# Attention preamble and first FFN tile: whole decay load, later bonus products, halved inverse scans, another order of DVE and ACT work

## The reference, cut

```python
def _attn_ref(r, k, v, w, u):              # B, H, S, D = 2, 8, 768, 48
    for t in range(S):
        kt, vt, rt, wt = (k[:, :, t], v[:, :, t], r[:, :, t], w[:, :, t])
        cur = np.einsum('bhd,bhe->bhde', u[None] * kt, vt)
        y[:, :, t] = np.einsum('bhd,bhde->bhe', rt, state + cur)
        state = wt[:, :, :, None] * state + np.einsum('bhd,bhe->bhde', kt, vt)
...
x = x @ w_in; x = where(x > 0, x, exp(min(x, 0)) - 1); x = x @ w_out    # 1536 x 384, 2048 wide
...
for e in range(4): out += p[:, e] * (relu(x @ w1[e]) @ w2[e])           # 1024 wide each
```

## Time and profile before

| | us |
|---|---|
| median of 3 runs | 662.99 (662.85 to 663.19) |
| the profiled execution, its own time | 663.25 |
| its span in the trace | 661.5 |
| PE busy in the span | 650.6 (98%) |
| DVE, ACT, POOL busy | 393.1, 238.0, 244.3 |

### The profile page before, as it was taken

One profiled execution on the slowest core, in us unless ns is written; L12 is line 12 of the kernel. 1 busy time (PEld: TensorE's weight loads), 2 busy tenths in 40 slices (PEclk: granted clock), 3 DMA queues, 4 the chain that ended last, 5 costly groups with the idle time before them and its releaser, 6 DMA issues.

```text
span 661.5 us, 12711 instructions
## 1 busy us (share of the span) xinstructions
PE 650.6 (98%) x4687; PEld 599.0 (91%) x4687; DVE 393.1 (59%) x717; ACT 238.0 (36%) x550; POOL 244.3 (37%) x292
## 2 busy tenths in 40 slices
PE   7998999999999999999999999999999999999998
PEld 5898999887778888999999999999999999999997
DVE  7878877765534333756565656565656565656563
ACT  4686655554445444422222222222222222222221
POOL 3898342221123079995007930008920009000000
PEclk9999999999999999999999999999999999999999
DMA  8923222220000033200002200003100011001011
GB/s 313 404 82 127 107 85 85 85 85 1 1 2 1 25 95 97 71 1 1 1 1 96 96 1 1 0 25 105 62 1 0 0 49 49 1 0 48 1 48 49
DMA packets 13423, 38.08 MB, mean 58 GB/s; under 512 B 1984, under 2 KB 4288, under 8 KB 13376
## 3 DMA queue, kind: packets, MB, share of 16 engines
q1 hardware_dynamic: 13088, 37.03, 16.0%
q10 hardware_dynamic: 288, 0.39, 0.2%
HBM read 35.06 MB, written 2.36 MB: 57 GB/s over the span
## 4 chain that ended last, share of the span: by engine, by line
PE 89%; DVE 3%; ACT 3%; issue 2%; DMA 1%; SPq 1%; DVEq 0%; ACTq 0%
PE bank L1143 28%; PE bank L1144 28%; PE bank L1145 28%; PE bank L1016 2%; DMA raw<-w_dram 1%; PE bank L1080 1%; ACT alpha L578 1%; PE bank L1039 1%; ACT neg L633 1%; PE bank L1027 1%; DVE st L784 1%; PE bank L1092 1%; ACT g_hi L641 0%; SPq L365 0%; DVE bank L845 0%
## 5 line engine op out<-in xcount | busy, mean ns | idle before, releaser
L1143 PE MATMUL bank<-x_lo,w_hi 128*128 128x256 f32 (+2 forms) x432 | 146.0, 338 | 0.9 <-DVE x_lo L809 0.9
L1145 PE MATMUL bank<-x_hi,w_hi 128*128 128x256 f32 (+2 forms) x432 | 143.3, 332 | 0.0
L1144 PE MATMUL bank<-x_hi,w_lo 128*128 128x256 f32 (+2 forms) x432 | 143.2, 331 | 0.0
L1144 PE MATMUL bank<-w_hi,g_lo 128*128 128x384 f32 x384 | 129.6, 338 | 0.0
L1145 PE MATMUL bank<-w_hi,g_hi 128*128 128x384 f32 x384 | 129.3, 337 | 0.0
L1143 PE MATMUL bank<-w_lo,g_hi 128*128 128x384 f32 x384 | 129.0, 336 | 0.0
L690 ACT ACTIVATE g_hi<-bank 128x512 fp32r<-128x512 f32 x96 | 57.6, 600 | 144.2 <-DVE bank L946 122.2
L1143 PEld LDWEIGHTS bank<-x_lo,w_hi 128*128 128x128 f32 x432 | 81.2, 188 | 10.0 <-POOL w_lo L470 1.0
L1145 PEld LDWEIGHTS bank<-x_hi,w_hi 128*128 128x128 f32 x432 | 81.2, 188 | 9.0
L1144 PEld LDWEIGHTS bank<-x_hi,w_lo 128*128 128x128 f32 x432 | 81.3, 188 | 8.3
L482 POOL TENSOR_TENSOR raw<-raw 128x128 f32<-128x128 f32 x16 | 7.4, 461 | 200.8 <-DMA raw<-w_dram 200.8
(11 more groups left out here) (111 smaller groups left out, 1146.1 us busy)
## 6 DMA issues: line engine op xcount, KB each, us to landing
raw<-w_dram SPq DMA_DIRECT2D x48, 384.0 KB, 3.6
rkw<-rkw_dram SPq DMA_DIRECT2D x10, 772.5 KB, 4.4
tok<-tok_dram SPq DMA_DIRECT2D x10, 576.0 KB, 6.1
out_dram<-acc SPq DMA_DIRECT2D x10, 192.0 KB, 1.9
rkw<-rkw_dram SPq DMA_DIRECT2D x2, 512.0 KB, 5.3
tok<-tok_dram SPq DMA_DIRECT2D x2, 192.0 KB, 5.5
out_dram<-acc ACTq DMA_DIRECT2D x2, 192.0 KB, 2.0
rkw<-rkw_dram SPq DMA_DIRECT2D x1, 260.5 KB, 5.2
```

Of the source, the lines that this page charges most:

```text
L1143: pe.matmul(out, wh, ml, start=start, stop=False, skip_group_check=shared)
L1144: pe.matmul(out, wl, mh, start=False, stop=False, skip_group_check=shared)
L1145: return pe.matmul(out, wh, mh, start=False, stop=stop, skip_group_check=shared)
```

## The change

- SP: the decays of chunk 0 come in one DMA, not in two halves; the two loads of u move ahead of the second decay load, and the constants behind it.
- DVE: the scan of chunk 0 is one instruction. `inverses(c)` for c >= 3 is cut into two halves of 260 columns, in steps 4c - 3 and 4c - 2, each between `elu` and `lo_g`. `add_update(c)` (c >= 2) goes from the end of step 4c + 3 to its beginning, ahead of `lo_x(c)`. The low part of slice 14 is made in steps 12 and 14, after `lo_g`.
- POOL: the product r*k of chunk 0 now waits for chunk 0's `scale_r`.
- ACT: `hi_x(1)` goes ahead of `hi_w(5)`; slice 6 is rounded inside step 0, the others follow a new table. `alphas`, `copy_tail`, `scale_state` come after the step's weight halves.
- PE: `values_odd(0)` goes ahead of `bonus(1)`.

```diff
-INVERSES = {c: step - 2 for c, step in SCORES.items()} | {FIRST: 3}
+INVERSES = {FIRST: 3}
+HALF_INVERSES = {c: step - 3 for c, step in SCORES.items() if c > FIRST}
...
-LO_BETWEEN = {1: (5, 0), 2: (5, 1), 3: (8, 0), 4: (8, 1), 6: (10, 0), 7: (10, 1), 14: (14, 1)}
-LO_AFTER = {10: (14, 0)}
+LO_BETWEEN = {1: (5, 0), 2: (5, 1), 3: (8, 0), 4: (8, 1), 6: (10, 0), 7: (10, 1)}
+LO_AFTER = {12: (14, 0), 14: (14, 1)}
...
-HI_FIRST = 7
-HI_BETWEEN = {0: ((7, 0), (7, 1)), 1: ((8, 0),), 2: ((8, 1),), 3: ((9, 0),), 4: ((9, 1),), 5: ((10, 0),), 6: ((10, 1),),
-              7: ((11, 0),), 8: ((11, 1), (12, 0)), 9: ((12, 1), (13, 0)), 10: ((13, 1), (14, 0)), 11: ((14, 1),),
-              12: ((15, 0),), 13: ((15, 1),)}
+HI_FIRST = 6
+HI_BETWEEN = {0: ((6, 0), (6, 1)), 1: ((7, 0),), 2: ((7, 1), (8, 0)), 3: ((8, 1),), 4: ((10, 0),), 5: ((10, 1),),
+              6: ((9, 0), (9, 1)), 7: ((11, 0),), 8: ((11, 1),), 9: ((12, 0), (12, 1)), 10: ((13, 0), (13, 1)),
+              11: ((14, 0), (14, 1)), 12: ((15, 0),), 13: ((15, 1),)}
...
-            load_decays(0, 0, SCAN // 2, s_half)
-            load_decays(0, SCAN // 2, RKW - 2 * NRK, s_first[0])
+            load_decays(0)
             load_rk(0)
-            sp.dma_start(const[:, :], const_d).then_inc(s_const, 16)
-            load_decays(1, 0, RKW - 2 * NRK, s_first[1])
             sp.wait_ge(s_zero, 1)
...
+            load_decays(1)
+            sp.dma_start(const[:, :], const_d).then_inc(s_const, 16)
             load_rk(1)
...
             for c in range(FIRST):
                 pool.wait_ge(s_rkw[c], 16)
-                if c > 0:
+                if c == 0:
+                    pool.wait_ge(s_qp, 1)
+                else:
                     pool.wait_ge(s_fr, c + 1)
...
-            for n in range(2, 5):
-                hi_w(n)
+            hi_w(2)
+            hi_w(3)
             hi_x(0, BANKS0["yt"])
+            hi_w(4)
+            hi_x(1, BANKS1["yt"])
             hi_w(5)
-            hi_w(6)
-            hi_x(1, BANKS1["yt"])
...
                 for c in due(n, 3):
+                    if c < NUPDATE:
+                        add_update(c, BESIDE)
                     lo_x(c, BESIDE["yt"])
                 elu(n)
...
+                for part in range(2):
+                    for c in due(n, part, HALF_INVERSES):
+                        inverses(c, part, 2)
                 for c in due(n, 0, SCALE_R):
...
-                for c in due(n, 3):
-                    if c < NUPDATE:
-                        add_update(c, BESIDE)
...
             values_even(0, BANKS0["yt"])
+            values_odd(0, BANKS0["yt"], s_val)
             bonus(1, BANKS1)
-            values_odd(0, BANKS0["yt"], s_val)
```

More of the change, by code:

```diff
@@ L94 @@
 PIECES = 4
-HI_FIRST = 7
-HI_BETWEEN = {0: ((7, 0), (7, 1)), 1: ((8, 0),), 2: ((8, 1),), 3: ((9, 0),), 4: ((9, 1),), 5: ((10, 0),), 6: ((10, 1),),
-              7: ((11, 0),), 8: ((11, 1), (12, 0)), 9: ((12, 1), (13, 0)), 10: ((13, 1), (14, 0)), 11: ((14, 1),),
-              12: ((15, 0),), 13: ((15, 1),)}
+HI_FIRST = 6
+HI_BETWEEN = {0: ((6, 0), (6, 1)), 1: ((7, 0),), 2: ((7, 1), (8, 0)), 3: ((8, 1),), 4: ((10, 0),), 5: ((10, 1),),
+              6: ((9, 0), (9, 1)), 7: ((11, 0),), 8: ((11, 1),), 9: ((12, 0), (12, 1)), 10: ((13, 0), (13, 1)),
+              11: ((14, 0), (14, 1)), 12: ((15, 0),), 13: ((15, 1),)}
+HI_HALVES = [half for step in sorted(HI_BETWEEN) for half in HI_BETWEEN[step]]
 WARM_UP = 5
@@ L292, in sums_of, with backwards @@
             return t[:, 0:FREE, :].rearrange("p s c -> p (s c)")[:, g % RING2 * SUMS * P:(g % RING2 + 1) * SUMS * P]
-        def backwards(t, first, row):
+        def backwards(t, first, row, count):
             full = t[:, :]
-            return bass.AP(full.tensor, first, [[row, P], [-1, SCAN]])
+            return bass.AP(full.tensor, first, [[row, P], [-1, count]])
         def factors(offset, half_step):
@@ L328, in hi_done @@
         def hi_done(n, part):
-            return 2 * n + part + 1
+            return 2 * n + part + 1 if n < HI_FIRST else 2 * HI_FIRST + HI_HALVES.index((n, part)) + 1
         def acc1(t, m):
@@ L385, in load_tok, with load_decays @@
                 sp.dma_start(tok[c % DEEP][:, :], tok_d[c]).then_inc(s_tok[c % DEEP], 16)
-            def load_decays(c, first, last, landed):
-                sp.dma_start(rkw[c][:, 2 * NRK + first:2 * NRK + last],
-                             rkw_d[c][:, 2 * NRK + first:2 * NRK + last]).then_inc(landed, 16)
+            def load_decays(c):
+                sp.dma_start(rkw[c][:, 2 * NRK:RKW], rkw_d[c][:, 2 * NRK:RKW]).then_inc(s_first[c], 16)
             def load_rk(c):
@@ L666, in _ @@
                     copy_kt(1, BANKS1)
-                for c in due(n, 0, ALPHAS):
-                    alphas(c)
-                    copy_tail(c)
-                for c in due(n, 0):
-                    scale_state(c)
                 for half in HI_BETWEEN.get(n, ()):
@@ L683, in _ @@
                         hi_x2(past, 2)
+                for c in due(n, 0, ALPHAS):
+                    alphas(c)
+                    copy_tail(c)
+                for c in due(n, 0):
+                    scale_state(c)
             def hi_relu(i, p, o):
@@ L734, in products, with inverses @@
                 need(dve, s_tail, c)
[L735 to L742 removed]
+                if c < FIRST:
+                    dve.wait_ge(s_first[c], 16)
+                dve.tensor_tensor_scan(fr[:, 0:SCAN], rkw[c % DEEP][:, 2 * NRK:2 * NRK + SCAN], reset[:, :], 0.0,
+                                       ALU.mult, ALU.add).then_inc(s_f, 1)
+                dve.wait_ge(s_f, c + 1)
                 dve.reciprocal(inv_end[:, SEG - 1:SCAN:SEG], fr[:, SEG - 1:SCAN:SEG]).then_inc(s_end, 1)
[L745 removed]
+            def inverses(c, part=0, parts=1):
                 dve.wait_ge(s_end, c + 1)
[L748 to L750 removed]
+                n = SCAN // parts
+                dve.tensor_tensor_scan(backwards(fr, 2 * SCAN - 1 - part * n, 2 * SCAN, n),
+                                       backwards(rkw[c % DEEP], 2 * NRK + SCAN - part * n, RKW, n),
+                                       backwards(inv_end, SCAN - 1 - part * n, SCAN, n), 0.0,
                                        ALU.mult, ALU.add).then_inc(s_fr, 1)
             def scale_k(c):
[L755 removed]
+                dve.wait_ge(s_fr, inverted(c))
                 landed(dve, s_rkw, c)
```

24 lines of the change are left out of this document (5 added, 19 removed).

## The result

The changed kernel takes 660.19 us (median of 5 runs, 660.10 to 660.32) against 663.19 us (median of 5 runs of the kernel before): a ratio of 0.9951, 95% interval 0.9936 to 0.9965. Its profiled execution took 660.15 us with a span of 658.4 us, 3.1 us under that of before. The forecast was 660.0 us and faster, so time and direction were right. The path to it was only in part: POOL let through 0.75 us more than forecast, and the places behind it took 0.6 us more than forecast. That the two nearly cancel is luck. Both profiled executions ran at a mean granted clock of 1.000, so their difference of 3.1 us owes nothing to TensorE's clock.

A forecast was written before the change was run, and what follows sets the result against it. Bound by a 20 us preamble chain, then PE with five stalls, POOL capping the gain. Terms 2.2 - 0.15 + 0.9 = 2.95 us off the 662.99 us median gave 660.0 us; range 658.8 to 661.3.

The forecast's parts named there:

- What bounds the kernel: Whole span: a 20 us preamble chained through DMA, DVE, PE and ACT, then PE with five stalls; about 11 us available.
- Loads, -0.3 us: Preamble: one DMA issue fewer, about 0.45 us, lets r and k of chunk 0 land 0.3 us earlier.
- Product off `scale_k(0)`, 1.09 gained, 0.7 lost: Preamble: scale_k(0) without POOL's product gains 1.09 us, chunk 1's inverse scan loses 0.7; with loads, scale_r(1) 0.7 us earlier.
- PE order and `hi_x(1)`, 1.1 and 0.54 us: Preamble: scores(1) starts 1.1 us earlier and hi_x(1) gains 0.54; first up gains 1.65 us.
- Stall at `scores(3)` gone: Step 13: scale_r(3), last needed, ends at 51.7 us before PE arrives at 52.2; PE would have 3.3 us.
- POOL as the cap, 1.1 us of wait: Slice 13 and turn_bonus(3): POOL lets through 2.2 of PE's 3.3 us; 1.1 us becomes a wait for POOL.
- POOL's row is 0.7 us earlier and no shorter: Steps 0 to 15: same POOL pieces beside the same scans, so slice 13 can gain 0.7 + 1.5 us.
- rival A: POOL takes less than granted, pieces meeting fewer DVE instructions or r and k landing 0.45 earlier: 658.9 us, chance 0.15.
- who queues behind the sum: Behind add_update(c) stand lo_x(c) and elu; elu waits 0.76 us for ACT anyway, so 0.73 us of adding fit.
- Step 17, -0.15 net: Chunk 4: 0.3 us gained from the state sum, 0.45 lost at down's third block through the half inverse ahead of lo_g.
- Chunks 5, 6, 7: 0.9 us: Steps 16 to 31: the state sum, 0.3 us late in each place, no longer holds PE; 0.9 us gained.
- ACT's order, nothing: ACT's steps: alphas and weight halves change places where elu is waited for anyway; booked at nothing.

The follow-up runs named there:

- the sum alone: Kernel before with only add_update(c) moved ahead of lo_x(c) and ELU in step 4c + 3: 662.31 us against 663.82, ratio 0.9979.
- the kernel with both fixes: Changed kernel with lo_x(3) ahead of add_update(3) and chunk 5's first half inverse behind the lo_x2 pieces in step 17: 659.89 us, ratio 0.9945.

## Why the prediction was right, and where it was not

- **What bounds the kernel.** Right: everything won is in PE's gaps, and PE's busy share rises from 98 to 99%.
- **Loads, -0.3 us.** Wrong in mechanism, harmless. r and k land 1.8 us earlier, not 0.3 (1.4 to 2.0 us, by the trace with the old loads that is taken, against the 4.94 us of this one). They stop being what `scale_k(0)` waits for, and the whole scan (3.64 us instead of a half at 3.03) leads instead: `scale_k(0)` starts 0.44 us earlier.
- **Product off `scale_k(0)`, 1.09 gained, 0.7 lost.** Measured 1.09 and 0.64, `scale_r(1)` 0.90 us earlier (0.7 forecast). As a row, right. Had POOL's product stood in the way in full, the loss would be 1.26 - 0.28 = 0.98 us and not the 0.8 of the forecast; the trace is under both. As a cause it fell: with the product not held back the time is the same.
- **PE order and `hi_x(1)`, 1.1 and 0.54 us.** Measured 0.99 (`scores(1)` is now behind `bonus(1)` on PE, 0.44 us after `scale_r(1)`) and 0.49; the first `up` gains 1.49 instead of 1.65.
- **Stall at `scores(3)` gone.** Right, with 3.23 us of lead for the 3.3 of the forecast. The last operand is ready earlier than it said: `scale_r(3)` ends at 49.50 us, not at 51.7. Of the reasons, the two pauses filled by halves were not needed there, and the 0.72 us of slice 14 is a compensation for ACT's table.
- **POOL as the cap, 1.1 us of wait.** The mechanism is right, its size is not: the wait is 0.28 us at slice 13. The step that failed is "POOL's row is 0.7 us earlier and no shorter". It is 1.58 us earlier at slice 13's second piece (0.89 from its start at 13.85 instead of 14.74, 0.7 from meeting DVE less). Undoing the halves gives 0.34 of it back; with ACT's order and the sum's place undone too, the piece starts at 52.18, another 0.14; the last 0.2 are the slices' new places by what is left over. The slack was also read 0.145 us too large, since PE starts that much after a piece ends. With both put right the sum closes: 1.58 + 1.52 - 0.145 = 2.95 us, the lead that was measured. So the first condition of rival A came true (the pieces meet fewer DVE instructions), but POOL did not let PE have all of it. The cap lay 0.75 us further out and still held.
- **`up(16)`.** Missing from the forecast. Its account of who queues behind the sum looked at `elu`, found about 0.75 us of slack there, and did not ask who waits for `lo_x(3)`. That low part is read by the first `up` of the second tile; scale (1.08 us beside POOL), sum and low part in a row end at 62.09, and 0.46 us of lead are lost. Putting `lo_x(3)` first gives 0.41 us of them back; the sum alone shows the wait purest, 0.80 us.
- **Step 17, -0.15 net.** Measured +0.21 at `scores(4)`, -0.49 at the third block. The forecast's -0.45 is nearly the sum, but not by its working: the half scan took 0.98 us (POOL beside it), not 0.65, and with it moved away the block starts only 0.33 us earlier. The other 0.15 us come, as the rows of the kernel with both fixes suggest, from the chain through ACT's step 15 and DVE's step 16, which the forecast didn't have.
- **Chunks 5, 6, 7: 0.9 us.** Measured 0.88 (2.21 to 3.09).
- **ACT's order, nothing.** Wrong, 0.65 us. The account of the change said that `alphas` and its companions come after the step's weight halves; they come after `hi_g` too, at the step's very end, and that is what counts.

Sum as measured: 2.95 - 0.46 + 0.21 - 0.49 + 0.88 = 3.09 us, against 2.2 - 0.15 + 0.9 = 2.95. POOL was 0.75 us kinder than forecast, and `up(16)` with step 17 took 0.6 us of that. The 3.09 us stand against one execution of before; by the medians the change is worth 2.8 us against the three first executions and 2.7 against those at full clock.

## What to carry to other kernels

When an instruction is moved ahead of others on an engine, list every reader of each one that it passes, not only the next link of the loop under study: in the kernel with the sum's move alone one late operand at a tile boundary made PE wait 0.80 us, more than the move had won up to there. On an engine that feeds two others (ACT here), the small work (here four activations on one column and a short copy) belongs behind the result that the others wait for; 1 us of it ahead of `hi_g` cost 0.65 us at the end. And a cap by another engine's row is only as good as the row's contents: if the change alters what runs beside it, the row's length has to be re-derived, since here it shrank by 0.7 us. And a wait that is missing from a list of waits may still be there: compare the starts of the same two instructions before and after, and look whether the distance from the suspected releaser is the same in every variant (here 0.145 us in nine traces).
